# Causal masks moved from TensorE's products to VectorE's minimum and Pool's selects, in an attention and two-expert-stage kernel

## What is computed

```python
scores = scale * np.matmul(q, k.transpose(0, 1, 3, 2))
cum = np.cumsum(np.log(np.clip(f, 0.0001, 1.0)), axis=-1)
decay = cum[:, :, :, None] - cum[:, :, None, :]
scores = np.where(causal, -1000000000.0, scores + decay)   # causal: k > q
scores = scores - np.max(scores, axis=-1, keepdims=True)
attn = np.exp(scores)
attn = attn / (np.sum(attn, axis=-1, keepdims=True) + 1e-09)
out = np.matmul(attn, v)
# then, for both expert stages
expert_idx = np.argmax(logits, axis=1)      # logits = cosine / tau, or x @ w_gate
h = np.maximum(x[mask] @ w1[e], 0.0)
out[mask] = gate_w[mask, None] * (h @ w2[e])
```

## Time and profile before

| | |
|---|---|
| Median of 3 runs | 971.01 us (966.63 to 971.33) |
| Profiled execution, own time | 969.89 us |
| Its span, first to last instruction | 968.3 us |
| TensorE matmul busy | 905.5 us, 94% |
| VectorE busy | 549.9 us, 57% |
| ScalarE busy | 403.2 us, 42% |
| Pool busy | 233.6 us, 24% |
| Mean granted TensorE clock | 0.963 of full speed |

### The profile page before, as it was taken

The page is one execution under the profiler, slowest core; times in us unless marked ns, Lnnn a source line. Parts: engine busy times, 40 slices in busy tenths (PEclk is TensorE's granted clock), DMA queues, the critical chain, the costliest instruction groups (busy, mean ns, idle before and its releaser), DMA issues.

```text
span 968.3 us, 16409 instructions
## 1 busy us (share of the span) xinstructions
PE 905.5 (94%) x5244; PEld 725.4 (75%) x5245; DVE 549.9 (57%) x1512; ACT 403.2 (42%) x708; POOL 233.6 (24%) x299
## 2 busy tenths in 40 slices
PE   6999999999989669999999999985999999999996
PEld 6677677666666558888888888874888888888885
DVE  6655657647556507847667776741666243526633
ACT  2444444454543305534525552521555252525532
POOL 6111122212210342323232323222222112222211
PEclk7999999999988869999999999996999999999998
DMA  5242342443521047616245554521666124616110
GB/s 145 68 120 71 113 119 80 148 130 97 163 85 55 26 144 264 207 42 213 92 141 171 185 169 141 170 71 27 206 208 217 45 96 158 207 39 207 45 34 22
DMA packets 59242, 119.64 MB, mean 124 GB/s; under 512 B 11934, under 2 KB 20638, under 8 KB 59204
## 3 DMA queue, kind: packets, MB, share of 16 engines
q1 hardware_dynamic: 49476, 96.90, 31.2%
q0 software_dynamic: 9440, 22.18, 7.0%
q10 hardware_dynamic: 288, 0.07, 0.0%
HBM read 104.14 MB, written 17.99 MB: 126 GB/s over the span
## 4 chain that ended last, share of the span: by engine, by line
PE 87%; ACT 4%; DVE 3%; DMA 3%; issue 2%; POOL 1%; SPq 0%; POOLq 0%; DVEq 0%; ACTq 0%
PE ps L587 26%; PE ps L558 26%; PE ps L415 7%; PE ps L428 7%; PE ps L423 4%; PE ps L378 3%; PE ps L381 3%; PE ps L395 3%; PE ps L396 2%; PE ps L433 2%; ACT qB L629 2%; PE ps L383 1%; PE ps L405 1%; PE ps L399 1%; ACT o_rows L637 1%
## 5 line engine op out<-in xcount | busy, mean ns | idle before, releaser
L975 DVE TENSOR_TENSOR wlo<-stage,whi 128x1024 fp32r<-128x1024 f32 x136 | 160.0, 1221 | 36.9 <-ACT whi L654 35.2
L654 ACT CAST whi<-stage 128x1024 fp32r<-128x1024 f32 x136 | 133.7, 1056 | 0.1
L720 ACT ACTIVATE h_s<-ps 128x512 f32<-128x512 f32 x44 | 26.3, 598 | 224.6 <-PE ps L558 224.6
L623 ACT ACTIVATE probT<-ps 128x576 f32<-128x576 f32 (+4 forms) x160 | 66.2, 434 | 125.1 <-PE ps L399 114.7
L415 PE MATMUL ps<-probT,v_s 128*65 128x448 f32 (+4 forms) x384 | 111.8, 402 | 0.0
L558 PE MATMUL ps<-whi,xT_hi 128*128 128x512 f32 x352 | 96.8, 398 | 3.0 <-DVE xT_lo L1029 3.0
L587 PE MATMUL ps<-whi,hT_hi 128*128 128x512 f32 x352 | 99.4, 404 | 0.0
L587 PE MATMUL ps<-whi,hT_lo 128*128 128x512 f32 x352 | 99.2, 403 | 0.0
L558 PE MATMUL ps<-wlo,xT_hi 128*128 128x512 f32 x352 | 96.6, 397 | 0.0
L558 PE MATMUL ps<-whi,xT_lo 128*128 128x512 f32 x352 | 96.5, 397 | 0.0
L395 PE MATMUL ps<-qB,kB 97*128 97x288 f32 (+2 forms) x192 | 87.7, 461 | 7.9 <-ACT qB L629 7.7
(11 more groups left out here) (181 smaller groups left out, 1562.8 us busy)
## 6 DMA issues: line engine op xcount, KB each, us to landing
stage<-in_moe_w SPq DMA_DIRECT2D x128, 512.0 KB, 4.5
q_raw<-in_q SPq DMA_DIRECT2D x64, 144.0 KB, 3.2
k_raw<-in_k SPq DMA_DIRECT2D x64, 144.0 KB, 3.1
v_s<-in_v SPq DMA_DIRECT2D x32, 162.5 KB, 2.3
x<-o_rows SPq DMA_DIRECT2D x8, 512.0 KB, 3.0
kB<-cum_hl SPq DMA_DIRECT2D x64, 2.2 KB, 1.7
table<-entry POOLq DMA_INDIRECT x44, 2.2
table<-tinit SPq DMA_DIRECT2D x2, 288.0 KB
```

What stands on the lines that cost most here:

```text
L623: act.activation(probT[0:M, PT_AT[t]:PT_AT[t] + S - t * P], ps[0:M, T_AT[t]:T_AT[t] + S - t * P], ACT.Exp, scale=-1.0).then_inc(exps_done, 1)
L654: act.copy(whi[b][:, c, :], stage[:, c, :]).then_inc(w_hi[c], 1)
L975: dve.tensor_tensor(wlo[b][:, c, :], stage[:, c, :], whi[b][:, c, :].bitcast(F32), ALU.subtract).then_inc(w_lo[c], 1)
```

## The change

`by_query` and `by_key` issue no mask product any more; the two products of a group are all there is. VectorE's minimum becomes one `tensor_tensor_reduce`, which adds a mask `maskf` (576 wide, zeros but for the last 128 columns, which hold 1e9 above the diagonal) to the PSUM tile, writes the tile back, and reduces with a minimum. In the transposed scores nothing is masked before the exponential; Pool sets the diagonal block's forbidden part of probT to zero (`clear`), and `weighted` waits for that and no longer for the exponential.

The order of TensorE's products changes: `back(h - 1)` moves from behind `by_key` 1 to ahead of the row product, `by_query` 3 moves ahead of `weighted` 0, and `weighted` 1 and 2 move back. VectorE takes `norm` last in a turn, `rest_k` earlier and `rest_q` later. Pool's copies are split, with selects between them. SP stores rows two heads later, ScalarE squares in heads 3 and 4, and the routing chain of a batch is cut in parts: the choice no longer waits for the scaling, the counts wait for `sum_done` and not for the whole entry, and the gate comes last. Warm-ups double, and Pool reads the number of tiles before it waits for the first table.

```diff
@@ SP
-                if h % HALF == 0 and h > 0:
-                    sp.wait_ge(norm_done, h)
-                    store_rows((h - 1) // H, (h - 1) % H // HALF)
+                if h % HALF == 2 and h > HALF:
+                    sp.wait_ge(norm_done, h - 2)
+                    store_rows((h - 3) // H, (h - 3) % H // HALF)
@@ TensorE, by_query
-                        mm = pe.matmul(o, qA[a][:, q0:q0 + P], kA[a][:, lo:hi], start=False, stop=not diag)
-                    if diag:
-                        mm = pe.matmul(ps[:, S_AT[j] + q0:S_AT[j] + q1], identb[:], maskb[:, 0:M], start=False, stop=True)
+                    mm = pe.matmul(o, qA[a][:, q0:q0 + P], kA[a][:, lo:hi], start=False, stop=True)
@@ TensorE, by_key
-                    if diag:
-                        M = min(P, S - k0)
-                        mm = pe.matmul(ps[:, col:col + M], maskb[:], identb[:, 0:M], start=False, stop=True)
@@ TensorE, turn h, as it is after the change
                 by_key(h, 0)
                 by_key(h, 1)
                 if more:
                     operands(n)
                     by_query(n, 4)
                 pe.wait_ge(exps_done, QT * h + 1)
                 by_key(h, 2)
...
                 if more:
                     by_query(n, 3)
                 pe.wait_ge(v_in[h % 3], (h // 3 + 1) * 16)
                 if h > 0:
                     pe.wait_ge(ot_done, h)
                 pe.wait_ge(cleared, QT * h + 1)
                 weighted(h, 0)
                 by_key(h, 3)
                 if more:
                     pe.wait_ge(mins_done, QT * n + 1)
                     by_query(n, 2)
                 pe.wait_ge(exps_done, QT * h + 2)
                 by_key(h, 4)
                 if more:
                     by_query(n, 1)
                     pe.wait_ge(mins_done, QT * n + 2)
                     by_query(n, 0)
                 pe.wait_ge(cleared, QT * h + 2)
                 weighted(h, 1)
                 if h > 0:
                     if more:
                         pe.wait_ge(mins_done, QT * (n + 1))
                     pe.wait_ge(s_embn, 3)
                     if h > 1:
                         pe.wait_ge(norm_done, h - 1)
                     back(h - 1)
                 if more:
                     pe.wait_ge(mins_done, QT * (n + 1))
                     minima_row(n)
...
                 weighted(h, 2)
...
                 weighted(h, 3)
...
                 weighted(h, 4)
                 if h % H == 6 and h > H:
                     pe.wait_ge(norm_done, h)
                     g_ranks(h // H - 1)
@@ TensorE, openings
-            pe.wait_ge(ent_done[0], B)
+            pe.wait_ge(sum_done, B)
             counts(0)
...
-                warm_up(WARM_UP if m else 2 * WARM_UP)
+                warm_up(WARM_UP * 2 if m else 4 * WARM_UP)
@@ ScalarE
                 exps(h, 0)
                 exps(h, 1)
+                exps(h, 2)
                 if h + 2 < HEADS:
                     leading_q(h + 2)
-                exps(h, 2)
...
+                    if hh == 3:
+                        act.wait_ge(norm_done, b * H)
+                        act.wait_ge(x1_stored, 64 * b)
+                        for t in range(3):
+                            g_square(b - 1, t)
+                    if hh == 4:
+                        for t in range(3, QT):
+                            g_square(b - 1, t)
+                    if hh == 6:
                         route_exp(b, b - 1)
-                if b == B - 1:
+                if b == B - 1 and hh < H - 1:
                     split_hi(0, hh, 1)
@@ VectorE, mins
-                dve.tensor_reduce(smin[0:q1 - q0, j:j + 1], ps[0:q1 - q0, S_AT[j]:S_AT[j] + q1], AX.X,
-                                  ALU.min).then_inc(mins_done, 1)
+                M = q1 - q0
+                tile = ps[0:M, S_AT[j]:S_AT[j] + q1]
+                at = S - P + M - q1
+                dve.tensor_tensor_reduce(out=tile, in0=tile, in1=maskf[0:M, at:at + q1], scale=1.0, scalar=LARGE, op0=ALU.add,
+                                         op1=ALU.min, accum_out=smin[0:M, j:j + 1]).then_inc(mins_done, 1)
@@ VectorE, turn h
-                if h > 0:
-                    norm(h - 1)
-                if n < HEADS:
-                    mins(n, 4)
                 if m < HEADS:
                     leading_k(m)
                 if n < HEADS:
+                    mins(n, 4)
                     mins(n, 3)
+                if m < HEADS:
+                    rest_k(m)
+                if n < HEADS:
                     mins(n, 2)
-                if m < HEADS:
-                    rest_q(m)
-                if n < HEADS:
                     mins(n, 1)
                     mins(n, 0)
                 if m < HEADS:
-                    rest_k(m)
+                    rest_q(m)
                 if h == 0:
                     embedding_rows()
+                else:
+                    norm(h - 1)
                 if b > 0 and hh == 5:
                     choose_batch(b - 1)
                 if b > 0 and hh == 6:
+                    scale_batch(b - 1)
                     read_ranks(b - 1)
-                    enter_batch(b - 1)
+                    place_batch(b - 1)
+                if b > 0 and hh == 7:
+                    gate_batch(b - 1)
@@ VectorE, after head 31
+            choose_batch(B - 1)
             dve.wait_ge(ssq_done, B)
             dve.wait_ge(sq_last, 1)
...
-            choose_batch(B - 1)
             read_ranks(B - 1)
-            enter_batch(B - 1)
+            place_batch(B - 1)
+            scale_batch(B - 1)
+            gate_batch(B - 1)
@@ Pool
+            def clear(h, t):
+                M = min(P, S - t * P)
+                block = probT[0:M, PT_AT[t]:PT_AT[t] + M]
+                pool.wait_ge(exps_done, QT * h + t + 1)
+                pool.affine_select(out=block, in_=block, compare_op=ALU.is_ge, fill=0.0, base=0, pattern=[[1, M]],
+                                   channel_multiplier=-1).then_inc(cleared, 1)
...
                 if h + 2 < HEADS:
-                    copies(h + 2)
-                if b > 0 and hh == 4:
+                    copy_k(h + 2)
+                clear(h, 0)
+                clear(h, 1)
+                clear(h, 2)
+                if h + 2 < HEADS:
+                    copy_q(h + 2)
+                clear(h, 3)
+                clear(h, 4)
+                if b > 0 and hh == 5:
                     norms(b - 1)
                 if b > 0 and hh == 7:
...
                     scatter(b - 1, range(0, 3))
```

More of the change, by code:

```diff
@@ L239, in get, with tile_loop @@
                 return self.eng.snap(v * times + plus) if (times, plus) != (1, 0) else v
-        def tile_loop(eng, m, e, body, split):
+        def tile_loop(eng, m, e, body, split, ready=None):
             n = eng.value_load(tiles_i[m][0:1, bass.ds(e, 1)], min_val=1, max_val=NRT)
+            if ready is not None:
+                ready()
             if split:
@@ L480, in _ @@
                 by_key(h, 1)
-                if h > 0:
-                    pe.wait_ge(ot_done, h)
-                    pe.wait_ge(s_embn, 3)
-                    if h % H == 7 and h > H:
-                        pe.wait_ge(rank_read, h // H)
-                    back(h - 1)
-                else:
-                    pe.wait_ge(s_embn, 1)
                 if more:
@@ L493, in _ @@
                 by_key(h, 2)
+                if more:
+                    if h == 0:
+                        pe.wait_ge(s_embn, 1)
+                    if h > 1:
+                        pe.wait_ge(norm_done, h - 1)
+                if h % H == 7 and h > H:
+                    pe.wait_ge(rank_read, h // H)
+                if more:
+                    by_query(n, 3)
                 pe.wait_ge(v_in[h % 3], (h // 3 + 1) * 16)
+                if h > 0:
+                    pe.wait_ge(ot_done, h)
+                pe.wait_ge(cleared, QT * h + 1)
                 weighted(h, 0)
@@ L503, in _ @@
                 pe.wait_ge(exps_done, QT * h + 2)
-                weighted(h, 1)
                 by_key(h, 4)
@@ L509, in _ @@
                     by_query(n, 0)
-                pe.wait_ge(exps_done, QT * h + 3)
-                weighted(h, 2)
+                pe.wait_ge(cleared, QT * h + 2)
+                weighted(h, 1)
+                if h > 0:
+                    if more:
+                        pe.wait_ge(mins_done, QT * (n + 1))
+                    pe.wait_ge(s_embn, 3)
+                    if h > 1:
+                        pe.wait_ge(norm_done, h - 1)
+                    back(h - 1)
                 if more:
@@ L884, in route_choose @@
                 io = iota8[:].unsqueeze(1).to_broadcast([P, g, E])
-                l, e = lg[:, lo:lo + g, :], eqi[:, lo:lo + g, :]
-                if m == 0:
-                    link(dve.tensor_tensor(l, raw, wide(rsc, lo, g), ALU.mult))
-                else:
+                l, e = (raw if m == 0 else lg[:, lo:lo + g, :]), eqi[:, lo:lo + g, :]
+                if m == 1:
```

(6 more changed lines are left out.)

150 lines of the change are left out of this document (71 added, 79 removed).

## The result

The changed kernel takes **944.66 us** (median of 4 runs, 937.10 to 949.29), the kernel before 969.4 (966.63 to 971.33). The ratio is 0.9739, 95% interval 0.9703 to 0.9775: 2.6% faster. Forecast: 942, range 928 to 962. The profiled execution took 944.56 us, its span is 943.0.

What follows compares the result with a forecast made beforehand. TensorE, busy 94% of the span, was taken as the bound. Masks 27, plus order 10, minus 17 for disturbances, plus 8 for tail and openings make 28 us off 969.9: 942, range 928 to 962.

Steps and rivals of the forecast that it cites:

- Order: Reordered TensorE products remove each head's waits for the row copy (0.28) and last minimum (0.05): 10 us over 31 heads.
- The tie: At the back products, TensorE is ready 5.3 us into a head and VectorE's minima chain ends at 5.25: level.
- Rival 1: The minima chain becomes the bound, 0.3 to 0.5 us a head, 9 to 15 us: 953; chance 0.16.
- Selects on Pool: Five per head, 0.28 to 0.35 us each, fitting a cover of 0.45; they cost nothing where Pool is free.
- (c): Routing work delays copy_k, the first select, g_ranks and route_exp in routing heads: 8.7 us in all.
- (a): Pool's three-tile table scatter stands ahead of copy_k and select at heads 16 and 24: 3.3 us lost twice, 6.6.
- (b): ScalarE's squares and hi-splits ahead of keep_ot and the first exponential: 2.3 us each in batches 1 and 2, 6.2 last.
- (d): About five low-clock spells (1.2 GHz) on TensorE in heads 18 to 31, some 1.7 us each: 8.5 us.
- Tail and openings: From head 31 on: 3.2 us from earlier entries and tile count, 2.5 and 2.2 from the two expert openings: 8.
- Rival 4: Fewer disturbances, with slack after the scatter and only two low-clock spells: 930; chance 0.12.
- Rival 2: The masked minimum on VectorE runs at two cycles per element, adding 41 us: 983, slower; chance 0.08.
- rival 3: Pool's and ScalarE's queues cost half as much again, with eight or more low-clock spells, 14 to 18 us: 958; chance 0.14.

Runs made afterwards that it cites:

- experiment 1: The kernel before with its ten mask products per head left out and nothing else changed; 945.38 us in one run, undisturbed heads 8.34 us.
- experiment 2: The changed kernel with ten zero-mask products per head put back on TensorE at their old places; 964.52 us, ratio 0.9951.
- experiment 4: The changed kernel with one more VectorE write of 128x256 ahead of the last minimum of each head; 952.05 us, ratio 0.9816.
- experiment 3: The changed kernel with Pool scattering one tile in each of five heads, behind that head's selects, instead of three and two; 924.85 us, ratio 0.9540.
- experiment 5: The changed kernel with scatters spread and only the first expert opening's warm-ups halved; 926.2 us, ratio 0.9556.
- experiment 8: The changed kernel with scatters spread and most of the next expert's weight loads held on SP's queue until the second gather is in; 928.64 us, ratio 0.9578.

## Why the prediction was right, point by point

That 942 came within 3 us of 944.66 is luck: masks and order gave 7 more than forecast, tail and openings 8 less, and the two cancel.

**The bound.** Right: the gain is TensorE's own stream and its gaps. Undisturbed heads came to 7.55, not 7.75.

**Masks, 0.88 a head, 27 us.** Right: 0.91 by putting them back, 0.84 to 0.95 by taking them away, 28 us.

**Order, 0.33 a head, 10 us.** Low: 0.51, 16 us. The 0.28 went as read. My 0.05 ahead of the row product was the small part; experiment 1's 0.21 there appears only once the masks are gone. What I hadn't priced is that weighted tiles 2, 3 and 4 in a row, without the row product between them and without an end of the stream behind them, take 0.22 less (experiment 2). No run isolates a single move of the new order.

**The minimum, 0.1 on top.** Right in size: 0.08 for the read, and 0.76 instead of 0.67 in all, from start to start. By the Trainium skill (VectorE: DVE Perf Modes, "Two Vector instructions with no wait between them") it had to be two instructions, and it is: the second has a row of its own, 0.14. My sentence that by this rule the cost would be near 0.19, and the sum 9 us worse, was wrong: the rule gives the count, not the price, and most of the read lies beside the minimum.

**The tie.** Right: experiment 4 shows no slack. Rival 1 was a matter of a tenth.

**Selects on Pool.** Right in undisturbed heads: three in 0.79 and pairs in 0.73, all hidden. Pool's qB copy went from 0.66 to 1.16 beside VectorE's rest_k, without harm. Besides the scatters, weighted tile 0 waited 0.76 and 0.85 for the select in the routing heads 14 and 15, as (c) has it, though the signs said "else none", and 0.80 in head 19, TensorE's timeline:

```profile
182.38 1.16 PE L406 MATMUL ps<-probT,v_s 128*65 128x128 f32 x4 [0.80 <-POOL probT L1143]
```

Head 19 takes 8.55, 1.0 more than an undisturbed one, with the clock at 1.00 throughout. VectorE's leading_k starts only at 180.81, 2.5 us behind the row copy instead of 1.0, and the q and k that it needs had been issued behind a weight load and the row stores, from 174.04 to 177.42. So the later row stores, which I put at nothing, seem to cost a head something where a weight load stands with them (head 11, behind row stores alone, takes 7.55); in experiment 3 it is 0.5. No run moves them alone.

**(a) Scatters, 3.3 each.** The mechanism and both places were right, 3.97 and 3.70 measured: 7.7 for 6.6.

**(b) and (c).** Right. Squares in batches 1 and 2: 1.42 and 0.8 over an undisturbed head, for 1.5 and 0.8; the routing heads behind them 0.93 and 1.83 together, for 2.6. The last batch came cheaper: in experiment 3, where neither a scatter nor the clock stands in between, its heads 24 to 30 are 7.1 over undisturbed ones, for 9.7. In the last four heads by_key 2 waited 2.15, 1.54, 0.34 and 1.76 for ScalarE.

**(d) The clock, five spells of 1.7, 8.5.** This is the step that was mis-sized. The price was carried over from spells behind small gaps to two full stops of 4 us, which cost 5.5 and 4.3 more. With 1.6 at head 28 (against the same head of experiment 3) the clock takes about 11.4 us, in three spells and not five. I should have asked what a stop that I had myself predicted would do to the clock; and as experiment 2 shows, even like stops are not followed by like spells. Over heads 1 to 30 the disturbances come to 37.4 where I had 34.5, with the clock 2.9 above my figure and the rest (7.7 for the scatters, 18.3 for all others, against 26) as forecast. The kernel before had 18.0 there, so 19.3 are lost where I said 17. The first head, whose distance to the next row copy fell from 11.71 to 8.95, gives 1.3 of it back, so that over all 31 heads it is 18.

**Tail and openings, 8 us.** Wrong: nothing came. The second opening gave more than forecast (21.2 to 17.3 from its warm-ups to the turn of h_s, 3.9 for 2.2), in this execution; with the same warm-ups it took 19.1 and 20.5 in those of experiments 5 and 8. The first gave nothing. Pool's root ended 17.7 us after the start of head 31 instead of 14.5, as its five scatters began 3.1 later than I had them, behind the earlier batch's gate on VectorE. The entries were done at 20.8, not 16.2: besides the 3.2 of the root, 1.4 come from VectorE's unexplained wait of 3.04 (experiment 5), without which the gate ends 1.7 behind the root in experiment 3, as forecast. And what the warm-ups saved in clock went into a wait for the second gather (2.83), which I never looked at, with another low-clock stretch behind it. From the last row copy to the turn of h_s at 338.04 it is 0.7 less than before, from there to the second opening 4.6 more: 3.9 - 4.6 + 0.7 is nothing.

Sum: 44 for masks and order instead of 37, 18 given back instead of 17, nothing instead of 8, less 0.8 at the start: 25 for 28. Rival 4 (fewer disturbances, 930) was what the placing of the scatters decided: with them spread it is 924.85. Rival 2 fell with the first row of L823. Of rival 3 neither half came: the queues cost what was counted, and there were three spells, though two of them long.

## What to carry to other kernels

A wait on a loaded TensorE can be priced twice: its own length, and the clock behind it, which here cost from nothing to 5.5 us, not always the same behind the same stop. Look for an in-order queue on which slow issues (a scatter, 1.0 plus 0.3 each) stand ahead of something that TensorE wants within 2 us, and spread them; where the wait can't go, harmless products in it kept the clock up here and saved the larger part (9.7 of 17.4). And follow a saving at an opening to the next transfer before counting it: here the time gained ahead of the first gather ended in a wait for the second.

## What the runs showed of the hardware that I had not expected

A stop of 4.3 us brought the granted clock down to 0.50 for twelve us of unbroken work, one of 3.75 us in experiment 2 for less than four, and 64 small products in its place kept it at 1.00. A stop of 2.15 us did so in some executions and in others not, at the same place of the same instructions. VectorE's masked minimum, with two operands and a written tile, runs at the pace of the plain reduction (0.77 against 0.756 us at 576 wide), and its accumulator read costs 0.08.
